# Two chunks and a semaphore inside an attention pair, and four zero tiles along the SP queue

## The reference

```python
# block-causal attention: B=4, H=8, S=576, D=64, blocks of 64
scores = where(block(i) >= block(j), q @ k.T / 8, -1e9)
x = softmax(scores) @ v                     # -> 2304 tokens x 512
# MoE with a skip: E=8 experts, 512 -> 1024 -> 512
out = x
for tokens with x @ w_skip > 0:  e = argmax(x @ w_gate)
    out += gate_w * (relu(x @ w1[e]) @ w2[e])
# dense MLP, 512 -> 2048 -> 512, all tokens
h = out @ w_in;  g = max(h, 0) + alpha * min(h, 0);  return g @ w_out
```

## Time and profile before

| | us |
|---|---|
| three timed runs | 853.64, 856.97, 862.86 (median 856.97) |
| the profiled execution | 853.48 |
| its span, first to last instruction | 851.6 |
| PE busy | 803.7 (94%) |
| DVE busy | 446.4 (52%) |
| POOL busy | 257.6 (30%) |
| ACT busy | 257.0 (30%) |

### The profile page before, as it was taken

The page is one execution under the profiler, slowest core; times in us unless marked ns, Lnnn a source line. Parts: engine busy times, 40 slices in busy tenths (PEclk is TensorE's granted clock), DMA queues, the critical chain, the costliest instruction groups (busy, mean ns, idle before and its releaser), DMA issues.

```text
span 851.6 us, 15189 instructions
## 1 busy us (share of the span) xinstructions
PE 803.7 (94%) x5137; PEld 699.8 (82%) x5138; DVE 446.4 (52%) x934; ACT 257.0 (30%) x621; POOL 257.6 (30%) x191
## 2 busy tenths in 40 slices
PE   6899999999579999999679999999999999999997
PEld 4677777777469898999569899989999999999996
DVE  4577777778854444234645744444444434444432
ACT  5465565565422313233311121112112112112111
POOL 7768668664011151015278810010001001000000
PEclk9899999999869999999879999999999999999999
DMA  6899999985419666168433120001002002001001
GB/s 159 193 219 246 233 234 258 251 208 168 117 51 331 212 208 235 37 198 319 147 104 109 50 71 3 0 16 58 0 0 74 0 0 74 0 0 37 1 1 37
DMA packets 94538, 99.16 MB, mean 116 GB/s; under 512 B 64048, under 2 KB 65200, under 8 KB 94000
## 3 DMA queue, kind: packets, MB, share of 16 engines
q1 hardware_dynamic: 85856, 70.89, 31.2%
q0 software_dynamic: 4208, 14.95, 6.0%
q10 hardware_dynamic: 4448, 13.01, 4.3%
HBM read 64.78 MB, written 20.19 MB: 100 GB/s over the span
## 4 chain that ended last, share of the span: by engine, by line
PE 88%; DVE 4%; DMA 4%; issue 2%; SPq 1%; ACT 1%; POOL 0%; DVEq 0%; POOLq 0%
PE bank L986 23%; PE bank L997 23%; PE bank L936 10%; PE bank L950 8%; PE bank L809 5%; PE bank L797 5%; PE bank L820 4%; PE bank L844 2%; PE bank L790 2%; PE bank L763 2%; DMA w_sb<-in_moe_w_dram 2%; PE bank L826 1%; PE bank L974 1%; PE bank L923 1%; PE bank L799 1%
## 5 line engine op out<-in xcount | busy, mean ns | idle before, releaser
L1517 DVE TENSOR_SCALAR g_sb<-bank,alpha_sb 128x384 f32<-128x384 f32 x96 | 59.3, 618 | 215.0 <-PE bank L986 214.8
L1177 ACT CAST g_hi<-g_sb 128x384 fp32r<-128x384 f32 x96 | 49.4, 514 | 322.5 <-DVE g_sb L1519 322.5
L986 PE MATMUL bank<-u_hi,wi_hi 128*128 128x384 f32 x384 | 130.1, 339 | 1.4 <-DVE u_lo L1490 1.4
L986 PE MATMUL bank<-u_hi,wi_lo 128*128 128x384 f32 x384 | 130.1, 339 | 0.0
L986 PE MATMUL bank<-u_lo,wi_hi 128*128 128x384 f32 x384 | 129.6, 338 | 0.0
L997 PE MATMUL bank<-wo_hi,g_hi 128*128 128x512 f32 x285 | 111.7, 392 | 1.8 <-DVE g_lo L1523 1.8
L997 PE MATMUL bank<-wo_lo,g_hi 128*128 128x512 f32 x285 | 112.6, 395 | 0.0
L997 PE MATMUL bank<-wo_hi,g_lo 128*128 128x512 f32 x285 | 112.3, 394 | 0.0
L1065 ACT ACTIVATE p_sb<-bank,neg_max 128x128 f32<-128x128 f32 (+2 forms) x144 | 79.4, 551 | 73.7 <-DVE neg_max L1217 70.0
L936 PEld LDWEIGHTS bank<-rows_t,w_sb 128*128 128x128 f32 x832 | 97.0, 195 | 2.6 <-DVE rows_t L1434 1.5
L936 PE MATMUL bank<-rows_t,w_sb 128*128 128x128 f32 x832 | 97.2, 279 | 1.1 <-DVE rows_t L1434 1.1
(11 more groups left out here) (176 smaller groups left out, 1204.3 us busy)
## 6 DMA issues: line engine op xcount, KB each, us to landing
w_sb<-in_moe_w_dram ACTq DMA_DIRECT2D x6, 2048.0 KB, 8.5
w_sb<-in_moe_w_dram SPq DMA_DIRECT2D x6, 2048.0 KB, 10.0
qk_t<-qk_t SPq DMA_DIRECT2D x30, 288.0 KB, 4.2
w_sb<-in_moe_w_dram SPq DMA_DIRECT2D x16, 512.0 KB, 5.6
y_slots<-zeros SPq DMA_DIRECT2D x6, 1024.0 KB, 5.6
qk_t<-qk_t SPq DMA_DIRECT2D x34, 144.0 KB, 3.3
v_nat<-in_v_dram SPq DMA_DIRECT2D x32, 128.0 KB, 3.4
y_out<-in_moe_w_out_dram POOLq DMA_DIRECT2D x16, 256.0 KB, 2.9
```

What stands on the lines that cost most here:

```text
L986: last = pe.matmul(dst, w[:, j, P * f:P * f + P], u[:, j, :], start=z == 0, stop=z == len(terms) - 1)
L1517: dve.tensor_scalar(g, a, 0.0, alpha_sb[:, f:f + 1], ALU.min, ALU.mult).then_inc(neg_done, 1)
```

## The change

Three edits, all in the attention stage:

1. On PE, chunk 1 (q) moves from behind `probs_t(4)` to behind the scores of unit 7, ahead of `probs_t(5)`. Scores of unit 7 so follow `probs_t(4)` directly. ACT's and DVE's orders and the ring stay as they are.
2. A new semaphore `x_main` is incremented by the third of the five matmuls of `to_rows`. The first operation of `x_out` (L1255) waits for it, and the wait for `x_tr` (all five) moves behind it.
3. Steps 1 to 4 of the SP queue no longer write a zero tile each. The addresses of the later ones move down by four tiles, and the last DMA of zeros, behind step 14, has eight tiles instead of four.

```diff
-        LAST_TILES = SLOT_TILES - KD - REST_TILES * (PAIRS - 3 - 2 * KD)
+        LAST_TILES = SLOT_TILES - REST_TILES * (PAIRS - 3 - 2 * KD)
...
                 if e:
                     save_tile(m - 1)
-                else:
-                    zero_tiles(m - 1, 1)
...
-                zero_tiles(KD + (n - 2 * KD - 1) * REST_TILES, REST_TILES)
+                zero_tiles((n - 2 * KD - 1) * REST_TILES, REST_TILES)
...
-            sp.wait_ge(y_zeroed, 16 * (PAIRS - 2 - KD))
+            sp.wait_ge(y_zeroed, 16 * (PAIRS - 2 - 2 * KD))
...
                     last = pe.matmul(to, o_t[:, P * i:P * i + P], w, start=True, stop=True)
+                    if i == IN_MAIN - 1:
+                        last.then_inc(x_main, 1)
                 last.then_inc(x_tr, 1)
...
-                    if c == QK_AT[0] + 1 and turns(n):
-                        qk_chunk(0, n + 2, par, ring("qk", 0, n))
+                    for j in range(2):
+                        if c == QK_AT[j] + 1 and turns(n):
+                            qk_chunk(j, n + 2, par, ring("qk", j, n))
                     probs_t(c, n)
...
-                        if j and at == c and turns(n):
+                        if j == 2 and at == c and turns(n):
                             qk_chunk(j, n + 2, par, ring("qk", j, n))
...
                 dve.wait_ge(inv_done, n + 1)
-                dve.wait_ge(x_tr, n + 1)
+                dve.wait_ge(x_main, n + 1)
...
                 dve.tensor_tensor(dst[:, 0:IN_MAIN], ...)
+                dve.wait_ge(x_tr, n + 1)
                 dve.tensor_tensor(dst[:, IN_MAIN], ...)
```

More of the change, by code:

```diff
@@ L304, in program @@
         o_evac = sem("o_evac")
+        x_main = sem("x_main")
         x_tr = sem("x_tr")
```

## The result

| | before | changed |
|---|---|---|
| median of five runs, us | 856.75 | 849.65 |
| lowest to highest | 853.64 to 862.86 | 849.45 to 852.48 |
| profiled execution (span) | 853.48 (851.6) | 852.48 (850.6) |

The ratio is 0.9936, with a 95% interval of 0.9907 to 0.9965: 3 to 8 us faster. The profiled execution of the changed kernel is its slowest of the five, and it shows a wait for a late transfer that is a sixth as long in a second profile of the same kernel (after_again, 849.56 us). The L numbers of the changed kernel differ from those of before by up to three: the chunks are L762, scores L796, transposes L808, `x_out` L1257, the low swap L461.

What follows compares the result with a forecast made beforehand. PE's own order was taken to bound attention's pairs 1 to 13, with the SP queue's transfers close beside it. Gains of 2.2 + 0.3 + 0.2 = 2.7 us, taken from 855.3, gave 852.6 us; range 848.5 to 858.5.

Steps and rivals of the forecast that it cites:

- PE's own order sets the time: Attention, pairs 1 to 13: PE's matmul order sets the 12.81 us period, so time removed from it is gained.
- more than the starts show: Rival: the hole ahead of the q chunk is 0.28 a pair and x_main gives 0.1; 849.9 us, chance 0.15.
- Edit 1, 2.2 us: Unit 7's scores fill PE's hole ahead of the q chunk: 0.17 us in each of 13 pairs, 2.2 us.
- The upper bound: Most the q chunk's move could gain, from the weight load's wait: 3.6 us, 0.28 in each of 13 pairs.
- Edit 2, 0.3 once, nothing in steady pairs: Earlier start of x_out: 0.3 us once, in pair 15's step 8; zero in steady pairs, bound 0 to 0.1 each.
- Edit 3, the cover for edit 1: Removing zero tiles from SP's steps 1 to 4 keeps swaps in time for the q chunk's gain; itself +0.2 us.
- at least 1.5: SP queue at step 5: of 4.4 us more lead and 0.9 less, at least 1.5 us was counted on.
- At or above the cover they had: Swaps in steps 5 to 8 keep their earlier cover, though the queue loses 4 x 0.35 = 1.4 us there.
- 2 MB of zeros at the end cost nothing: Zeros behind step 14 take some 11.2 us; pair 15's v still lands with 3.2 us cover, cost zero.
- The sum of 2.7 us: Whole-kernel gain: 2.2 for the q chunk, 0.3 for x_main and 0.2 for the late swap.
- Slower: Rival: removed zeros do not speed up SP, and swaps come late in steps 5 to 8; 860.5 us, chance 0.10.
- The signs: Right: no L763 wait, x_out 12.6 us apart. Wrong: period stays 12.8, or PE waits for L460 in pairs 5 to 9.

Runs made afterwards that it cites:

- after_again: The changed kernel unaltered, timed and profiled once more against the kernel before; median 849.67 us, ratio 0.9946.
- before_again: The kernel before, unaltered, profiled once more; 855.12 us in one execution.
- zeros_in_5_to_8: The changed kernel with its four moved zero tiles in steps 5 to 8, not behind step 14; 853.62 us, ratio 0.9995 against the kernel before.
- two_swaps_early: As first_swap_early, with step 1's low swap also ahead of its loads and the router's weights between pair 1's swaps; 844.93 us, ratio 0.9877 against before.
- first_swap_early: Changed kernel with steps 5 to 8's saves behind step 14 and pair 1's first swap ahead of pair 3's q and k loads; 846.40 us, ratio 0.9880 against before.
- q_alone: The kernel before with only the move of the q chunk; 854.48 us, ratio 1.0001.
- x_main_alone: The kernel before with only the new semaphore x_main; 857.63 us in one execution.

## Why the prediction was right, point by point

- *PE's own order sets the time*: right. The hole went and the pair is shorter by what it was.
- *The number*: 852.6 was forecast and 849.65 measured, inside the range. But the gain was 5.5 us by the ratio and 7.1 by the medians, against 2.7 in the sum; the range was wide enough for the spread of the times, and so for this too. The rival "more than the starts show" had named 849.9.
- *Edit 1, 2.2 us*: the mechanism was right and the term was mis-sized. 0.26 a pair over 13 pairs is 3.4. The step that failed is the one that took the matmuls' starts, and not the load's wait of 0.28, for the size of the hole. The upper bound was nearly the value. The rule of the Trainium skill ("Perfetto Trace Analysis", "Identifying the Most-Contended Engine") to go by the weight load and not by matmul time, as the prediction applied it to the hole, gave 3.6; the measured period agrees with it (0.26 a pair against 0.28) and not with my choice of 0.17.
- *Edit 2, 0.3 once, nothing in steady pairs*: right, it is 0.4. From the start of `to_rows` to the first operation of `x_out` it is 1.15 us (216.29 to 217.44) instead of 1.51 (216.62 to 218.13), so 0.36 was gained there and not the 0.29 of the idle.
- *Edit 3, the cover for edit 1*: right in kind, and shown: neither edit alone gives anything that can be measured. The reading of the earlier trace rows, that a swap put down to ACT was late by its landing, held up: with edit 3 alone that pair went from 13.00 to 12.80. The lead at step 5 was there: the low swap is issued at 78.93 for a unit 0 at 86.72, 7.8 us of cover against 5.8 before, and "at least 1.5" was right. What the queue loses behind it was wrong. I let it lose 0.35 a step in steps 5 to 8, from 12.99 against 12.64. In the changed kernel those steps start at 74.02 and end at 128.24, 13.56 each, against 12.55: 1.0 a step. So the lead is used up at step 9's swap, and it was late there in both profiles. "At or above the cover they had" was false (4.0 us at step 9 and 4.8 in after_again, against 5.5 there before). Why the same bytes took 12.99 a step before and 13.56 here is open.
- *2 MB of zeros at the end cost nothing*: right. The last pairs are 12.30 and 11.78 us long, and the wait for v is not there.
- *The sum of 2.7 us*: the terms that were measured give 3.4 + 0.4 = 3.8 for two undisturbed executions, and 228.21 to 223.91 is 4.3 with the 0.2 of the swap at 88.97. But 1.6 of the 4.3 stand already at the first `x_out` (40.28 to 38.71), where the two profiles of before differ by 0.4 from each other, so the agreement is in part luck. The two ratios say 5.5 and 4.6; I take the difference for late swaps and the later stage, in executions of before like before_again; that share was not measured by itself. I had priced an execution of before that was nearly undisturbed, and so missed that part.
- *The rivals*: "more than the starts show" came true in its first half (the load's wait, not x_main's 0.1). "Slower" had the right place for a late swap, but its condition, that the zeros do not speed up SP, did not hold, and neither did its price: the late swap of 1.7 us cost 3.6 with its clock in one profile, and 0.5 in the other.
- *The signs*: the wait at L763 is gone, the period is 12.55 and the idle ahead of `x_out` 0.3, as said. But a sign of being wrong came as well: the changed profile has PE waits for the low swap in pairs 7 and 9 (0.23 and 1.74 us). And "attention ends 2.7 us earlier" is 0.7 in the first profile (228.21 to 227.50) and 4.3 in the second.

## What to carry to other kernels

Here a queue and an engine ran within two per cent of each other, and a gain on the engine was worth nothing until the queue was lightened, and the other way round. In such a case try the two edits together, and each alone, before judging either. Judge a hole in TensorE's stream by the wait of its weight load and by the period of the loop; the distance between matmul starts showed 0.17 of the 0.26 here. In a full queue count the time from issue to PE's turn against the landing at every step, not on average: what is urgent is decided by its place, and writes that nobody waits for belong behind the last urgent transfer.

## What the runs showed of the hardware

- The length of a wait alone does not tell whether the granted clock falls behind it. In the changed kernel a wait of PE of 1.74 us was followed by 0.72 over six us and cost as much again as the wait; waits of 1.07 (before_again), 1.98 (zeros_in_5_to_8) and 2.46 us (two_swaps_early) left it at 1.00, and one of 2.66 (first_swap_early) was followed by 0.57 over 3.3 us.
- The same 2 MB load, at the same place of the program, took from 9.9 to 15.0 us in kernels that differ only in attention; two of the longest three came with edits that leave the order of the DMAs alone (q_alone 15.0, x_main_alone 14.5). This was not expected, and its cause is open.
